# Whole-pair loads of q, k and v, q and k turned by products with the identity, in a fused attention and two-layer kernel

## The reference

```python
k_sum = k.reshape(B, H, nb, block, D).max(axis=3)
v_sum = v.reshape(B, H, nb, block, D).mean(axis=3)
scores_all = np.concatenate([where(mask_l, scale*q@k.T, -1e9), scale*q@k_sum.T + log(block)], -1)
x = softmax(scores_all) @ concatenate([v, v_sum])
```

## Time and profile before

| | |
|---|---|
| median of 3 runs | 538.21 us (536.62 to 539.1) |
| the profiled execution: its own time, its span | 538.56 us, 536.8 us |
| mean granted TensorE clock | 0.978 |
| PE / DVE / ACT / POOL busy | 502.4 / 235.5 / 212.6 / 112.3 us |
| attention (first to last score) | about 9 to 116 us |

### The profile page before, as it was taken

One profiled execution on the slowest core, in us unless ns is written; L12 is line 12 of the kernel. 1 busy time (PEld: TensorE's weight loads), 2 busy tenths in 40 slices (PEclk: granted clock), 3 DMA queues, 4 the chain that ended last, 5 costly groups with the idle time before them and its releaser, 6 DMA issues.

```text
span 536.8 us, 8565 instructions
## 1 busy us (share of the span) xinstructions
PE 502.4 (94%) x3312; PEld 420.5 (78%) x3312; DVE 235.5 (44%) x625; ACT 212.6 (40%) x433; POOL 112.3 (21%) x100
## 2 busy tenths in 40 slices
PE   3698879897999999999999999999999999999997
PEld 2476657675779889899988888888888888888885
DVE  2445644652684255455256454423233333333231
ACT  2346634751574346345455443324121223222222
POOL 2263838440012002002445353200000000000000
PEclk9999965999899999999999999999999999999999
DMA  9579596934000000017000000002000002000002
GB/s 176 115 137 229 130 216 147 227 118 206 0 0 2 1 0 1 1 45 269 1 1 0 1 0 2 0 1 78 1 0 0 1 0 78 0 0 0 0 0 78
DMA packets 46402, 30.35 MB, mean 57 GB/s; under 512 B 40096, under 2 KB 40096, under 8 KB 45472
## 3 DMA queue, kind: packets, MB, share of 16 engines
q1 hardware_dynamic: 46368, 29.89, 21.6%
HBM read 25.17 MB, written 3.15 MB: 53 GB/s over the span
## 4 chain that ended last, share of the span: by engine, by line
PE 80%; DMA 5%; SPq 4%; POOL 4%; DVE 3%; ACT 2%; issue 2%; DVEq 0%; POOLq 0%
PE bank L854 12%; PE bank L856 12%; PE bank L855 12%; PE bank L1056 8%; PE bank L1057 8%; PE bank L1055 8%; PE bank L1011 4%; PE bank L1013 4%; PE bank L1012 4%; DMA vblocks<-in_v 3%; PE bank L931 2%; POOL vblocks L406 2%; SPq L311 2%; PE bank L997 2%; PE bank L898 1%
## 5 line engine op out<-in xcount | busy, mean ns | idle before, releaser
L615 ACT ACTIVATE ex<-bank 128x512 f32<-128x512 f32 x48 | 28.7, 598 | 127.9 <-PE bank L856 127.9
L856 PE MATMUL bank<-yt_lo,w2in_hi 128*128 (+1 forms) x192 | 74.7, 389 | 0.0
L855 PE MATMUL bank<-yt_hi,w2in_lo 128*128 (+1 forms) x192 | 74.7, 389 | 0.0
L1055 PE MATMUL bank<-w2out_hi,g_hi 128*128 128x512 f32 x192 | 74.7, 389 | 0.0
L1056 PE MATMUL bank<-w2out_lo,g_hi 128*128 128x512 f32 x192 | 74.7, 389 | 0.0
L854 PE MATMUL bank<-yt_hi,w2in_hi 128*128 (+1 forms) x192 | 74.7, 389 | 0.0
L1057 PE MATMUL bank<-w2out_hi,g_lo 128*128 128x512 f32 x192 | 74.7, 389 | 0.0
L832 DVE TENSOR_SCALAR ex<-ex 128x512 f32<-128x512 f32 x48 | 21.6, 450 | 116.5 <-ACT ex L615 116.5
L837 DVE TENSOR_TENSOR g_lo<-gf,g_hi 128x512 fp32r<-128x512 f32 x48 | 46.5, 969 | 35.9 <-ACT g_hi L623 35.9
L623 ACT ACTIVATE g_hi<-gf 128x512 fp32r<-128x512 f32 x48 | 30.3, 632 | 49.0 <-DVE gf L834 49.0
L498 ACT ACTIVATE se<-se,nm 128x120 f32<-128x120 f32 x96 | 32.5, 387 | 36.4 <-DVE nm L683 36.4
(11 more groups left out here) (103 smaller groups left out, 845.1 us busy)
## 6 DMA issues: line engine op xcount, KB each, us to landing
w2in_raw<-in_w_in SPq DMA_DIRECT2D x1, 4096.0 KB, 12.3
w2out_raw<-in_w_out SPq DMA_DIRECT2D x4, 1024.0 KB, 9.4
kraw<-in_k SPq DMA_DIRECT2D x16, 192.0 KB, 5.3
qraw<-in_q SPq DMA_DIRECT2D x16, 192.0 KB, 4.0
vblocks<-in_v SPq DMA_DIRECT2D x4, 768.0 KB, 8.8
out<-osb SPq DMA_DIRECT2D x12, 256.0 KB, 2.1
vw<-in_v SPq DMA_DIRECT2D x16, 176.0 KB, 6.1
win_raw<-in_w_in SPq DMA_DIRECT2D x4, 512.0 KB, 6.1
```

The source lines that it names most:

```text
L855: pe.matmul(acc, al, bh, start=False, stop=False)
L856: last = pe.matmul(acc, ah, bl, start=False, stop=(i == n - 1))
L1055: pe.matmul(dst, g_hi[:, j % GS, cols], w2out_hi[:, j, :], start=(j == 0), stop=False)
```

## The change

k and q of a pair come by one transfer each: partition p gets three successive tokens of each half of each head, a run of 768 bytes, where it was one token of 256 bytes. Four slots (`RAWS`) take the place of two. As the tokens of a partition are no longer 128 apart, `turn_heads` turns them by 12 products with the identity per pair and tensor (64 columns of weights, 128 columns streamed) and writes every third column of PSUM, starting at column 128 so that no half crosses a bank. They take the place of six transposes. V comes by one transfer into partitions 16 to 79, by head and then by tile (256-byte runs as before), and the halo by two. In SP's list the loads stand further ahead, the halo ahead of the means at the start, and the part of `w_in` or `w_out` of iteration n behind `move_means(n/2+1)`.

```diff
@@ -117,15 +117,18 @@
-        (kt, qraw), a1 = place(W2IN, ("kt", [P, 2, HALO + S + HALO], F32), ("qraw", [P, 2, T, P], F32))
+        RAWS = 4
+        (kt, kraw, qraw), a1 = place(
+            W2IN, ("kt", [P, 2, HALO + S + HALO], F32), ("kraw", [P, RAWS, 2 * HALVES, TG * D], F32),
+            ("qraw", [P, RAWS, 2 * HALVES, TG * D], F32))
         assert a1 <= XY
...
         (vblocks,), _ = place(3 * KD * F1 * 4, ("vblocks", [NB * HPM, 2, BLOCK * D], F32))
-        (kraw, vw, qt, se, pt, vmean, ks, mt, mask, bands, xn), a2 = place(
-            LN, ("kraw", [P, 2, T, P], F32), ("vw", [P, VS, SUBS, 2, D1], F32),
+        (vw, qt, se, pt, vmean, ks, mt, mask, bands, xn), a2 = place(
+            LN, ("vw", [P, VS, 2, SUBS, D1], F32),
             ("qt", [P, 2, S], F32), ("se", [P, RING, 2, KEYS], F32),
@@ -162,8 +165,8 @@
         pool_step = sem("pool_step")
-        k_loaded = [sem("k_loaded0"), sem("k_loaded1")]
-        q_loaded = [sem("q_loaded0"), sem("q_loaded1")]
+        k_loaded = [sem(f"k_loaded{i}") for i in range(RAWS)]
+        q_loaded = [sem(f"q_loaded{i}") for i in range(RAWS)]
         v_loaded = [sem("v_loaded0"), sem("v_loaded1"), sem("v_loaded2")]
@@ -246,8 +249,7 @@
-        V_DMAS = 4
-        REST = S - HALO - (SUBS - 1) * SUB
+        HALO_DMAS = 2
         T_LAG, PV_LAG, X_LAG = 2, 3, 6
@@ -260,22 +262,18 @@
         def _(sp):
-            def pair_of_heads(x, n):
-                return x[2 * n:2 * n + 2].rearrange("h (t p) d -> p t h d", p=P)
+            def thirds(x, n):
+                return x[2 * n:2 * n + 2].rearrange("h (f p i) d -> p (h f) (i d)", p=P, i=TG)
             def load_k(n):
-                if n >= 2:
-                    sp.wait_ge(kv_in_psum, n - 1)
-                for h in range(2):
-                    sp.dma_start(kraw[:, n % 2, :, h * D:(h + 1) * D],
-                                 pair_of_heads(kf, n)[:, :, h, :]).then_inc(k_loaded[n % 2], 16)
+                if n >= RAWS:
+                    sp.wait_ge(kv_in_psum, n - RAWS + 1)
+                sp.dma_start(kraw[:, n % RAWS, :, :], thirds(kf, n)).then_inc(k_loaded[n % RAWS], 16)
             def load_q(n):
-                if n >= 2:
-                    sp.wait_ge(q_in_psum, n - 1)
-                for h in range(2):
-                    sp.dma_start(qraw[:, n % 2, :, h * D:(h + 1) * D],
-                                 pair_of_heads(qf, n)[:, :, h, :]).then_inc(q_loaded[n % 2], 16)
+                if n >= RAWS:
+                    sp.wait_ge(q_in_psum, n - RAWS + 1)
+                sp.dma_start(qraw[:, n % RAWS, :, :], thirds(qf, n)).then_inc(q_loaded[n % RAWS], 16)
@@ -284,20 +282,17 @@
                     sp.wait_ge(attn_done, T * (n - VS + 1))
-                for h in range(2):
-                    body = vf[2 * n + h, HALO:HALO + (SUBS - 1) * SUB, :].rearrange("(j i) d -> i j d", i=SUB)
-                    sp.dma_start(vw[2 * HALO:LOCAL, s, 0:SUBS - 1, h, 0:D], body).then_inc(v_loaded[s], 16)
-                sp.dma_start(vw[HALO:2 * HALO, s, 0, :, 0:D],
-                             vf[2 * n:2 * n + 2, 0:HALO, :].rearrange("h i d -> i h d")).then_inc(v_loaded[s], 16)
-                sp.dma_start(vw[2 * HALO:2 * HALO + REST, s, SUBS - 1, :, 0:D],
-                             vf[2 * n:2 * n + 2, S - REST:S, :].rearrange("h i d -> i h d")).then_inc(v_loaded[s], 16)
+                sp.dma_start(vw[HALO:HALO + SUB, s, :, :, 0:D].rearrange("i h j d -> i (h j) d"),
+                             vf[2 * n:2 * n + 2].rearrange("h (j i) d -> i (h j) d", i=SUB)).then_inc(v_loaded[s], 16)
...
                 s = n % VS
-                sp.wait_ge(v_loaded[s], 16 * V_DMAS * (n // VS + 1))
-                sp.dma_start(vw[0:2 * HALO, s, 1:SUBS, :, :],
-                             vw[SUB:LOCAL, s, 0:SUBS - 1, :, :]).then_inc(halo_filled[s], 16)
+                if n == 0:
+                    sp.wait_ge(zeros_ready, 2)
+                sp.wait_ge(v_loaded[s], 16 * (n // VS + 1))
+                sp.dma_start(vw[0:HALO, s, :, 1:SUBS, :], vw[SUB:SUB + HALO, s, :, 0:SUBS - 1, :]).then_inc(halo_filled[s], 16)
+                sp.dma_start(vw[SUB + HALO:LOCAL, s, :, 0:SUBS - 1, :], vw[HALO:2 * HALO, s, :, 1:SUBS, :]).then_inc(halo_filled[s], 16)
@@ -317,38 +312,46 @@
+            def load_win(i):
+                sp.dma_start(win_raw[:, i, :], w_in[i * P:(i + 1) * P, :]).then_inc(win_loaded[i], 16)
+            def load_wout(i):
+                sp.dma_start(wout_raw[:, 2 * i:2 * i + 2, :],
+                             w_out[2 * i * P:(2 * i + 2) * P, :].rearrange("(k p) n -> p k n", p=P)
+                             ).then_inc(wout_loaded[i], 16)
             load_k(0)
+            load_vblocks(0)
             load_q(0)
-            load_vblocks(0)
             load_v(0)
             load_k(1)
+            fill_halo(0)
             move_means(0)
-            fill_halo(0)
             load_q(1)
+            load_v(1)
+            load_vblocks(1)
+            load_k(2)
+            load_q(2)
             for n in range(PAIRS):
+                if n + 1 < PAIRS:
+                    fill_halo(n + 1)
+                if n + 2 < PAIRS:
+                    load_v(n + 2)
                 if n % 2 == 0 and n // 2 + 1 < MEANS:
-                    load_vblocks(n // 2 + 1)
-                if n + 1 < PAIRS:
-                    load_v(n + 1)
-                if n + 2 < PAIRS:
-                    load_k(n + 2)
-                    load_q(n + 2)
+                    move_means(n // 2 + 1)
+                if n % 2 == 0 and n // 2 + 2 < MEANS:
+                    load_vblocks(n // 2 + 2)
+                if n + 3 < PAIRS:
+                    load_k(n + 3)
+                    load_q(n + 3)
...
                 if n < KD:
-                    i = n
-                    sp.dma_start(win_raw[:, i, :], w_in[i * P:(i + 1) * P, :]).then_inc(win_loaded[i], 16)
+                    load_win(n)
                 if n >= 4:
-                    i = n - 4
-                    sp.dma_start(wout_raw[:, 2 * i:2 * i + 2, :],
-                                 w_out[2 * i * P:(2 * i + 2) * P, :].rearrange("(k p) n -> p k n", p=P)
-                                 ).then_inc(wout_loaded[i], 16)
-                if n + 1 < PAIRS:
-                    fill_halo(n + 1)
-                if n % 2 == 0 and n // 2 + 1 < MEANS:
-                    move_means(n // 2 + 1)
+                    load_wout(n - 4)
@@ -433,7 +436,7 @@
                 pool.tensor_copy(vw[LOCAL:KEYS, s, :, :, 0:D],
-                                 mt[LOCAL:KEYS, c, None, i:i + 2, :].broadcast_to([NB, SUBS, 2, D])
+                                 mt[LOCAL:KEYS, c, i:i + 2, None, :].broadcast_to([NB, 2, SUBS, D])
                                  ).then_inc(means_spread, 1)
@@ -483,13 +486,13 @@
                     act.wait_ge(scores_in_psum, T * (n - 1))
-                act.activation(kt[:, n % 2, HALO:HALO + S], psQK[:, 0:S], ACT.Copy).then_inc(kt_ready, 1)
+                act.activation(kt[:, n % 2, HALO:HALO + S], psQK[:, P:P + S], ACT.Copy).then_inc(kt_ready, 1)
...
                     act.wait_ge(scores_in_psum, T * (n - 1))
-                act.activation(qt[:, n % 2, :], psQ(n)[:, 0:S], ACT.Copy).then_inc(q_copied, 1)
+                act.activation(qt[:, n % 2, :], psQ(n)[:, P:P + S], ACT.Copy).then_inc(q_copied, 1)
@@ -657,8 +660,8 @@
-            dve.memset(vw[:, :, 0, :, 0:D], 0.0)
-            dve.memset(vw[:, :, SUBS - 1, :, 0:D], 0.0).then_inc(zeros_ready, 1)
+            dve.memset(vw[0:HALO, :, :, 0, 0:D], 0.0)
+            dve.memset(vw[SUB:P, :, :, SUBS - 1, 0:D], 0.0).then_inc(zeros_ready, 1)
             dve.memset(kt[:, :, 0:HALO], 0.0)
@@ -856,31 +859,37 @@
+            def turn_heads(dst, rows, s):
+                for f in range(HALVES):
+                    for i in range(TG):
+                        for h in range(2):
+                            cols = dst[h * D:(h + 1) * D, P + f * GT:P + (f + 1) * GT].rearrange("d (p i) -> d i p", i=TG)
+                            last = pe.matmul(cols[:, i, :], rows[:, s, h * HALVES + f, i * D:(i + 1) * D], ident[:, :],
+                                             start=True, stop=True)
+                return last
             def prep_k(n):
-                s = n % 2
-                pe.wait_ge(k_loaded[s], 32 * (n // 2 + 1))
+                s = n % RAWS
+                pe.wait_ge(k_loaded[s], 16 * (n // RAWS + 1))
                 if n == 0:
...
                     pe.wait_ge(xlo_ready, 2 * n - 4)
-                for t in range(T):
-                    last = pe.transpose(psQK[:, t * P:(t + 1) * P], kraw[:, s, t, :], ident[:, :])
-                last.then_inc(kv_in_psum, 1)
+                turn_heads(psQK, kraw, s).then_inc(kv_in_psum, 1)
             def prep_q(n):
-                s = n % 2
+                s = n % RAWS
                 if n == 0:
...
                     pe.wait_ge(xlo_ready, 2 * n - 3)
-                pe.wait_ge(q_loaded[s], 32 * (n // 2 + 1))
```

(9 more changed lines are left out.)

## The result

The changed kernel takes 554.45 us (553.55 to 556.9), the kernel before in the same session 538.65 us: a ratio of 1.0299 with a 95% interval of 1.0244 to 1.0354. It is slower by some 16 us, and outside the range.

The account below looks back on a forecast made before the run. PE bounds attention, working or waiting for transfers. Pair 6 starts 0.9 us later and the last turn adds 0.7 us: +1.6 us on the profiled 538.56 us gives 540.2 us, as median 539.8 us; range 531 to 547 us.

Parts of the forecast that it names:

- the loop: SP waits for POOL's sum, POOL for the weight part issued behind the moves; pair 6 placed at 102.5 us, 9.5 later.
- the landing: In attention, a w_in part arrives 6.6 us after SP issues it, w_out part 0 after 5.5 us.
- B: Rival: weight parts land 3 to 3.6 us sooner, pair 6 is placed at 92 us; about 532 us; chance 0.27.
- The sum from there: PE starts pair 6 at 104.0 us, 0.9 us later; q's last turn adds 0.7 us: +1.6 us.
- Waits for k go: PE's waits of 0.8, 1.5 and 3.3 us for k and the halo vanish, as loads lie further ahead.
- The turns: On PE, each turn of k or q costs 0.7 us more at 2.4 GHz, 1.4 us more at 1.2 GHz.
- Rival C: Strided products on PE are twice as dear, 14.3 us a fast pair, +14 us, 552 us; chance 0.13.
- The clock: After PE idles 4.5 us before pair 4 the clock falls; 11.4 us at 1.2 GHz lose 0.38 of their length.
- D: Rival: PE's idle stretch brings 19.5 us at 1.2 GHz, or a second one: 543 us, up to 546; chance 0.20.
- A: Main case: the SP and POOL loop takes what loads give, -2 to +3 us, 536 to 541 us; chance 0.40.

Follow-up runs that it names:

- e5: The changed kernel with the next chunk for the means issued behind the weight part instead of ahead of k, q and it: 557.59 us.
- e12: The changed kernel, its order of loads kept, with POOL instead of SP issuing the moves of chunks 1 to 3: 534.22 us.
- e10: The changed kernel with e3's order of loads and POOL instead of SP issuing the moves of chunks 1 to 3: 532.78 us.
- e3: The changed kernel with k, q and the weight part issued ahead of the moves of the means, only the chunk behind: 536.82 us.
- e9: e3 with the halo of pair n+2 also filled ahead of the moves of the means: 536.97 us.
- e4: The changed kernel with k and q loaded and turned as before (two transfers of 256-byte runs, six transposes), four slots kept: 561.67 us.
- e7: e3 with k and q loaded and turned as before (two transfers of 256-byte runs, six transposes): 548.76 us.
- e6: The changed kernel with every turn of k and q done twice, 24 products in place of 12: 556.54 us.

## Why the prediction was wrong

- **What bounds the kernel, and the loop**: right. The rows show it as forecast: POOL idle before the even weight parts, then PE before pairs 2, 4 and 6. The first sum ended at 31.6 us (forecast 31.5), PE's first product with V came at 18.9 us (19.0), the parts were issued 6.0, 4.8 and 4.3 us behind the sum (6.1, 5.0, 4.4), split and placing took 5.0 us.
- **The step that failed is the landing**, a term of the sum: "6.6 us at the lesser". It measured 48.20 - 37.60 = 10.6 us, 80.66 - 70.42 = 10.2 us and 110.05 - 103.12 = 6.9 us (forecast 5.5). I took the value from rows in which V, k and q went ahead of the part, and in neither of them a chunk. In the new list the chunk of 768 KB goes right ahead of the first two even parts. I had even named it, against B, and gave it no price. e5 shows it: with the chunk behind the part the same landings took 8.2 and 6.8 us, and the third, which has no chunk ahead in either kernel, took 6.9 and 7.2 us. Whether SP's long wait also delays the landing by itself, as it leaves the DMA engines idle (a share of 0.05 from 32 to 36 us) and then sends 2 MB at once, is not shown. It isn't needed for a landing of that size: in e12, where SP does not wait, this part landed at 43.76 us, 11.8 us after its issue:

```profile
31.94 4.83 SPq L316 DMA_DIRECT2D win_raw<-in_w_in  x1
```

I had named the landing as the unknown and given ends of 2.8 and 9.4 us; even the upper end was too low, and the range did not carry it. The three landings are 4.0, 3.6 and 1.4 us over their terms. The waits for the odd parts, which I had taken as landed, add 1.5 and 2.2 us: the first was issued only at 48.07 us and landed 6.6 us later. So pair 2 came 4.0 us late, pair 4 9.0 us, pair 6 12.5 us: 115.0 us for 102.5 us.
- **The sum from there**: PE took up pair 6 at 115.29 us instead of 103.12 us, 12.2 us later (forecast 0.9). From there to the end of attention it lost 2.2 us more: 0.7 us for the turn of q, as forecast, and the rest in the slow clock behind that wait.
- **"Waits for k go"**: wrong. k of pairs 3 and 5 still made PE wait 3.49 and 1.79 us, which the prediction had listed as a sign of being wrong. Three pairs ahead is ahead of pairs, not of SP's wait.
- **The turns**: right to 0.1 us: 1.53 us fast, 2.83 us slow, for a forecast of 0.7 and 1.4 us above 0.85 and 1.54 us. Rival C and, with it, the Trainium skill's warning of strided PSUM patterns ("SBUF — State Buffer", section "Door 1: The DMA port swizzle") are not borne out here: with the stride of 12 bytes a column took 0.43 ns (last section), against the 0.48 ns that I had worked out for the products with V, which write without a stride.
- **The clock**: I gave the idle stretch before pair 4 11.4 us at 1.2 GHz behind it, 4.3 us of the sum. It was 3.4 us: the turn of q at 86.91 us took 2.83 us, and the product with V at 90.08 us 0.45 us again. The other idle stretches had up to 6 us behind them, as the last section shows for one. What hid this error was the larger one.
- **The rivals**: B had the sign of the landing wrong; D had the right side for a wrong reason. C's price is written wrongly: 2.1 us is more than a turn before, not more than in A, and its 14.3 us a pair follow from that. None had a late landing with a price, though the loop hung on it three times: 3.5 us more in each landing would have added some 10 us to the sum, 550 us.

## What to carry to other kernels

A queue that issues in program order and waits for a compute engine holds back all that stands behind it; before an item moves behind such a wait, look for who must have it before the engine can go on. If the wait closes a ring, its round time counts once per turn, and the landing in it has to be priced from a row with the same load ahead of it. Here it was better to let the producing engine issue the transfer of its own result (e10, e12; 2.06 to 2.27 us of POOL per chunk) than to reorder around the wait (e3, e9).

## What the runs showed of the hardware that I had not expected

**The clock came back sooner in the kernel whose turns are products.** Windows of the changed kernel around its second idle stretch (as the earlier trace rows):

```profile
48.00:52.00 4.00, 0.28 (x2) 0.04 (x1) 1.80 (x7) 0.98 (x4) 3.65 (x3) 1.00 1.10 305
52.00:56.00 4.00, 2.56 (x36) 2.42 (x38) 0.49 (x4) 0.59 (x2) 2.44 (x3) 0.53 0.98 171
56.00:60.00 4.00, 4.00 (x52) 2.98 (x48) 0.55 (x5) 1.20 (x4) 3.86 (x3) 0.61 0.04 4
60.00:64.00 4.00, 3.99 (x75) 3.09 (x71) 2.46 (x13) 2.75 (x8) 3.84 (x3) 1.00 0.02 4
```

After 5.16 us of idle PE the clock was back at 2.4 GHz some 6 us after work resumed at 53.4 us, with one turn of q in between; before, with transposes, it took 19.5 us. This agrees with the Trainium skill, "TensorE: Matmul & The Clock Gate", section "Part 4: PE-mode transpose", by which transposes do not count as busy as products do, and with the mean clocks of the runs of e4 (0.926 to 0.947, against 0.957 to 0.971 of the changed kernel), e7 (0.938 to 0.965, against 0.978 to 0.987 of e3) and e6 (0.975 to 0.988). None of the three changes the turns without the transfers or the amount of work, so it is not shown apart.

**A turn by products streams at half the time per column of a transpose**: 24 instructions of 128 columns, on two column groups by turns, add 1.31 us at 2.4 GHz (2.84 - 1.53 in e6), 0.43 ns a column; six transposes of 128 columns stream 0.7 us, 0.9 ns a column. Twelve products have four times the columns, and so cost twice the time.
